# First expert's rows gathered by quarters and turned by VectorE, on one core of a Trainium2

## What is computed

```python
x = attention(q, k, v)                               # 2304 rows of 512
x = (sigmoid(x @ w_gate) * (x @ w_val)) @ w_out      # hidden size 1536
logits = x @ g + log1p(exp(x @ g_noise)) * noise     # 8 experts
top2, weight = two best experts of a row, softmax of the two
for e in range(8):                                   # hidden size 1024
    out[rows of e] += weight * (relu(x[rows of e] @ w1[e]) @ w2[e])
```

## Time and profile before

| | |
|---|---|
| median of 3 runs | 974.71 us (974.69 to 976.02) |
| the profiled execution | 974.4 us |
| its span, first to last instruction | 972.5 us |
| TensorE busy | 963.2 us, 99%, 6467 products |
| VectorE, ScalarE, GpSimd busy | 516.2, 372.1, 424.5 us |
| granted TensorE clock | 0.998 |
| the first expert's TensorE turns (L1097) | 20 transposes, 3.0 us busy |

### The profile page before, as it was taken

One profiled execution on the slowest core, in us unless ns is written; L12 is line 12 of the kernel. 1 busy time (PEld: TensorE's weight loads), 2 busy tenths in 40 slices (PEclk: granted clock), 3 DMA queues, 4 the chain that ended last, 5 costly groups with the idle time before them and its releaser, 6 DMA issues.

```text
span 972.5 us, 17622 instructions
## 1 busy us (share of the span) xinstructions
PE 963.2 (99%) x6467; PEld 847.9 (87%) x6467; DVE 516.2 (53%) x1285; ACT 372.1 (38%) x892; POOL 424.5 (44%) x417
## 2 busy tenths in 40 slices
PE   9999999999999999999999999999999999999997
PEld 7998888888888888888999899898998989898995
DVE  6565576765757576574546633444443434444430
ACT  6553343433333343422344423343434334343411
POOL 4882224242332434232215453664828284664402
PEclk9999999999999999999999999999999999999999
DMA  6756333343533325232134163672736465473503
GB/s 227 233 173 165 119 110 108 96 138 97 142 106 125 99 75 152 76 100 87 44 121 133 30 156 79 169 161 84 156 77 146 100 151 129 118 163 75 98 3 52
DMA packets 85335, 113.64 MB, mean 117 GB/s; under 512 B 20800, under 2 KB 48448, under 8 KB 85248
## 3 DMA queue, kind: packets, MB, share of 16 engines
q1 hardware_dynamic: 71376, 85.18, 30.0%
q0 software_dynamic: 13584, 27.05, 13.9%
q10 hardware_dynamic: 288, 0.26, 0.1%
HBM read 83.69 MB, written 28.77 MB: 116 GB/s over the span
## 4 chain that ended last, share of the span: by engine, by line
PE 98%; ACT 1%; DVE 0%; issue 0%; POOL 0%; POOLq 0%; DVEq 0%
PE bank L1129 22%; PE bank L1113 22%; PE bank L1018 16%; PE bank L1041 16%; PE bank L1024 11%; PE bank L1022 5%; PE bank L998 2%; PE bank L936 2%; PE bank L1136 1%; PE bank L1067 1%; PE bank L1077 0%; PE bank L954 0%; ACT arena L1268 0%; PE bank L1097 0%; POOL out L816 0%
## 5 line engine op out<-in xcount | busy, mean ns | idle before, releaser
L1024 PE MATMUL bank<-xr,wr 128*128 128x256 f32 x864 | 242.6, 281 | 0.0
L1018 PE MATMUL bank<-xr,wr 128*128 128x512 f32 x672 | 239.9, 397 | 0.0
L1113 PE MATMUL bank<-wr 128*128 128x256 f32 (+1 forms) x1536 | 223.4, 306 | 0.3 <-DVE wr L1748 0.3
L1113 PEld LDWEIGHTS bank<-wr 128*128 128x128 f32 x1536 | 221.2, 190 | 2.0 <-DVE wr L1748 0.7
L798 POOL DMA_INDIRECT arena<-x_rows,shared x128 | 139.8, 1092 | 131.2 <-DVE v_nat L1735 88.4
L763 POOL TENSOR_TENSOR hr<-arena,hr 128x256 fp32r<-128x256 f32 x84 | 62.0, 738 | 263.5 <-ACT hr L1319 263.5
L1041 PE MATMUL bank<-wr,hr 128*128 128x512 f32 x648 | 170.6, 398 | 0.0
L1024 PEld LDWEIGHTS bank<-xr,wr 128*128 128x128 f32 x864 | 163.6, 189 | 3.5
L1018 PEld LDWEIGHTS bank<-xr,wr 128*128 128x128 f32 x672 | 126.2, 188 | 30.2
L1041 PEld LDWEIGHTS bank<-wr,hr 128*128 128x128 f32 x648 | 114.0, 188 | 23.7 <-issue 0.6
L1129 PE MATMUL bank<-wr 128*128 128x512 f32 (+1 forms) x576 | 132.6, 390 | 0.0
(11 more groups left out here) (161 smaller groups left out, 1013.6 us busy)
## 6 DMA issues: line engine op xcount, KB each, us to landing
arena<-moe_w SPq DMA_DIRECT2D x36, 512.0 KB, 3.7
arena<-moe_w SPq DMA_DIRECT2D x112, 128.0 KB, 3.4
p_rows<-arena SPq DMA_DIRECT2D x28, 256.0 KB, 2.0
v_nat<-p_rows SPq DMA_DIRECT2D x112, 64.0 KB, 2.0
arena<-gv SPq DMA_DIRECT2D x12, 512.0 KB, 4.5
out<-zeros POOLq DMA_DIRECT2D x20, 256.0 KB, 2.8
x_rows<-arena SPq DMA_DIRECT2D x9, 512.0 KB, 3.9
arena<-k SPq DMA_DIRECT2D x17, 256.0 KB, 4.2
```

Source lines behind the costliest of these rows:

```text
L1018: pe.matmul(ps_g[m].rearrange("p (a n) -> p a n", a=2), gv_w[:, f, m, kk], xr[:, g % 2, :, kk], start=(kk == 0), stop=False, skip_group_ch ...
L1024: mm = pe.matmul(ps_g[m][:, 0:GT], gv_w[:, f, 2 + m, kk], xr[:, g % 2, 0, kk], start=False, stop=(kk == KC - 1), skip_group_check=True)
L1113: mm = pe.matmul(ps_h[u % 2][:, 0:n], w1_r[e % 2][:, a, kk, f * P:(f + 1) * P], xT[p][:, b, kk, 0:n], start=(kk + x == 0), stop=(kk == KC ...
```

## The change

It makes the first expert's tiles squared like all others. TensorE's `turn_g` goes, and its calls: three in slots 104 to 106 (n = 0, 1, 2) and two in `up(1, 0, f)` behind f = 4 and 6 (n = 6, 7). VectorE turns them: n = 0 at the end of slot 103, n = 1 in slot 104, n = 2 in slot 106, n = 6 behind f = 3, n = 7 behind f = 5. The high and low parts of n = 0, 1, 2 are made in slots 104, 105 and 107 (before: 104, 105, 106). GpSimd issues four DMAs for each of the five tiles. The first expert's w1 is loaded in quarters. The table `tab_q_first` holds both experts and takes eight DMAs; VectorE waits for it in slot 100 (before: slot 103). A new table `tab_q_next` for n = 6, 7 takes four DMAs ahead of `tab`; VectorE waits for it ahead of `hidden_low(1, 0, 0)`. `tab_q` holds all eight experts. Gather 7 is issued ahead of the second scatter. Apart from this, in the last group's choice `hidden_low(0, 0, 5)` stands behind the first three instructions rather than behind the first eight.

```diff
+    FIRST_ROWS = [LAST - 4, LAST - 3, LAST - 1]
...
-        def turned_at(n):
-
-            return x_t if squared(n) else ps_xt.rearrange("p (k m) -> p k m", k=KC)
...
         def gathers(n):
 
-            return 16 * sum(4 if squared(i) else 1 for i in range(n % 2, n + 1, 2))
+            return 64 * ((n - n % 2) // 2 + 1)
...
-                if n < KC and e >= SQUARES:
+                if n < KC:
 
                     for j in range(4):
                         sp.dma_start(raw[j * Q4:(j + 1) * Q4, n % 4], w1_q[e, j, n]).then_inc(raw_e[n % 4], 16)
...
-                    for j in range(4):
-                        sp.dma_start(tab_q_first[j * Q4:(j + 1) * Q4].rearrange("p b n w -> p b (n w)"),
-                                     places.rearrange("(b c e n) w -> c b e (n w)", b=4, c=Q4, e=NE)[:, :, SQUARES, 0:2 * HEAD]
-                                     ).then_inc(tab_q_first_in, 16)
+                    for e in range(AHEAD):
+                        for j in range(4):
+                            sp.dma_start(tab_q_first[j * Q4:(j + 1) * Q4, e].rearrange("p b n w -> p b (n w)"),
+                                         by_quarter[:, :, e, 0:2 * HEAD]).then_inc(tab_q_first_in, 16)
...
             sp.wait_ge(placed_late, 16 * 2 * CH * (GROUPS - EARLY))
+            for j in range(4):
+                sp.dma_start(tab_q_next[j * Q4:(j + 1) * Q4].rearrange("p b n w -> p b (n w)"),
+                             by_quarter[:, :, 0, 2 * HEAD:2 * TILES]).then_inc(tab_q_next_in, 16)
             sp.dma_start(tab[:].rearrange("p n w -> p (n w)"), places.rearrange("(p n) w -> p (n w)", p=P)).then_inc(tab_in, 16)
...
-                if n == AHEAD * HEAD:
-                    pool.wait_ge(tab_in, 16)
...
-                if squared(n):
-                    if n == HEAD:
-                        pool.wait_ge(quarters_first, 1)
...
+                if n == 0:
+                    pool.wait_ge(quarters_first, 1)
+                if n == AHEAD * HEAD:
+                    pool.wait_ge(quarters_next, 1)
+                if n == AHEAD * HEAD + LATE:
+                    pool.wait_ge(quarters_done, 1)
...
             gather(6)
+            gather(7)
             scatter(1)
-            gather(7)
             scatter(2)
...
-                if LAST - 4 <= s < LAST - 1:
-                    turn_g(s - (LAST - 4))
...
             for f in range(F2C):
                 up(1, 0, f)
-                if f in (4, 6):
-                    turn_g(f // 2 + 4)
...
-                if LAST - 4 <= s < LAST - 1:
-                    xt_high(s - (LAST - 4))
+                if s in FIRST_ROWS:
+                    xt_high(FIRST_ROWS.index(s))
...
                 relu(1, 0, f)
-                if f in (4, 6):
-                    xt_high(f // 2 + 4)
+                if f in (3, 5):
+                    xt_high(6 + (f - 3) // 2)
...
+                if s == LAST - 8:
+                    dve.wait_ge(tab_q_first_in, 16 * 4 * AHEAD)
+                    link(dve.tensor_scalar(quarter[:], quarter[:], 5, None, ALU.arith_shift_right))
+                    to_quarters(tab_q_first[:].rearrange("p e b n w -> p (e b n) w")[:, :, 0]).then_inc(quarters_first, 1)
                 if s == LAST - 5:
-                    dve.wait_ge(tab_q_first_in, 16 * 4)
...
-                if LAST - 4 <= s < LAST - 1:
-                    xt_low(s - (LAST - 4))
+                    turn_rows(0)
+                if s in FIRST_ROWS:
+                    xt_low(FIRST_ROWS.index(s))
+                if s == LAST - 4:
+                    turn_rows(1)
+                if s == LAST - 2:
+                    turn_rows(2)
...
             hidden_low(0, 0, 4)
-            choose_first(GROUPS - 1)
+
+            add_noise(GROUPS - 1)
             hidden_low(0, 0, 5)
+            choose(L[:], marks[:, 0], top[:, 0])
             choose_second(GROUPS - 1)
...
             low(1, HEAD)
+            dve.wait_ge(tab_q_next_in, 16 * 4)
+            to_quarters(tab_q_next[:].rearrange("p b n w -> p (b n) w")[:, :, 0]).then_inc(quarters_next, 1)
             for f in range(F2C):
                 hidden_low(1, 0, f)
...
-                if f in (4, 6):
-                    xt_low(f // 2 + 4)
+                if f == 3:
+                    turn_rows(6)
+                if f == 4:
+                    xt_low(6)
+                if f == 5:
+                    turn_rows(7)
+                    xt_low(7)
```

More of the change, by code:

```diff
@@ L135, in attention_two_moe_program @@
         noise_s = shared[:, 3 * WIN:].rearrange("p (t e) -> p t e", e=NE)
-        tab_q = shared[:, 0:8 * (NE - SQUARES) * TILES].bitcast(I32).rearrange("p (b e n w) -> p b e n w", b=4, n=TILES, w=2)
+        tab_q = shared[:, 0:8 * NE * TILES].bitcast(I32).rearrange("p (b e n w) -> p b e n w", b=4, n=TILES, w=2)
         zeros = sb("zeros", [P, P])
@@ L176, in attention_two_moe_program @@
         quarter = sb("quarter", [P, 1], I32)
-        tab_q_first = sb("tab_q_first", [P, 4, HEAD, 2], I32)
+        tab_q_first = sb("tab_q_first", [P, AHEAD, 4, HEAD, 2], I32)
+        tab_q_next = sb("tab_q_next", [P, 4, LATE, 2], I32)
         idx_r = sb("idx_r", [P, 1], I32)
@@ L350, in attention_two_moe_program @@
         quarters_first = sem("quarters_first")
+        tab_q_next_in = sem("tab_q_next_in")
+        quarters_next = sem("quarters_next")
         quarters_done = sem("quarters_done")
@@ L380, in attention_two_moe_program @@
         ORDER = [0, 1, 2, 5, 6, 7, 3, 4, 8, 9] + list(range(AHEAD * TILES, ALL))
-        def turned_at(n):
-            return x_t if squared(n) else ps_xt.rearrange("p (k m) -> p k m", k=KC)
         def turn_no(m):
             return ORDER.index(m)
-        def squared(n):
-            return ORDER[n] // TILES >= SQUARES
         def loads(q):
-            return 16 * sum(4 if i // UNITS >= SQUARES and i % UNITS < KC else 1 for i in range(q % 4, q + 1, 4))
+            return 16 * sum(4 if i % UNITS < KC else 1 for i in range(q % 4, q + 1, 4))
         def gathers(n):
-            return 16 * sum(4 if squared(i) else 1 for i in range(n % 2, n + 1, 2))
+            return 64 * ((n - n % 2) // 2 + 1)
         def is_early(m):
@@ L524, in _ @@
         def _(sp):
+            by_quarter = places.rearrange("(b c e n) w -> c b e (n w)", b=4, c=Q4, e=NE)
             def load_k(t):
@@ L788, in gather @@
                     pool.wait_ge(xt_turned, n - 1)
-                if squared(n):
-                    if n == HEAD:
-                        pool.wait_ge(quarters_first, 1)
[L792 to L800, removed]
-                pool.nop(nofuse=True)
-                pool.indirect_dma_start(x_g[:, n % 2], None, x2_rows[:, :], bass.IndirectOffsetOnAxis(row_no(m), 0)
-                                        ).then_inc(gathered[n % 2], 16)
+                if n == 0:
[4 more added lines that the diff above has]
+                    pool.wait_ge(quarters_done, 1)
+                pool.nop(nofuse=True)
+                e, a = divmod(m, TILES)
+                for b in range(4):
+                    if is_early(m):
+                        no = tab_q_first[:, e, b, a, 0:1]
+                    elif e == 0:
+                        no = tab_q_next[:, b, a - HEAD, 0:1]
+                    else:
+                        no = tab_q[:, b, e, a, 0:1]
+                    pool.indirect_dma_start(x_g[:, n % 2, b * P:(b + 1) * P], None, x2_quarters,
+                                            bass.IndirectOffsetOnAxis(no, 0)).then_inc(gathered[n % 2], 16)
             def scatter(m):
@@ L1089, in rank_rows @@
                 pe.matmul(ps_rank, tri[:], chosen[:], start=False, stop=True, skip_group_check=True).then_inc(ranked, 1)
[L1091 to L1098, removed]
             def up(e, p, f):
@@ L1383, in xt_high @@
                     act.wait_ge(hr_used, LAST)
-                act.copy(xT[p][:, 0, :, cols], turned_at(n)).then_inc(xt_hi, 1)
+                act.copy(xT[p][:, 0, :, cols], x_t).then_inc(xt_hi, 1)
             def relu(e, p, f):
@@ L1666, in choose_first, with add_noise @@
             def choose_first(g):
+                add_noise(g)
+                choose(L[:], marks[:, 0], top[:, 0])
+            def add_noise(g):
                 dve.wait_ge(soft, 3 * g + 2)
@@ L1731, in turn_rows @@
                 dve.wait_ge(gathered[n % 2], gathers(n))
-                dve.wait_ge(xt_hi, n)
-                dve.wait_ge(xt_lo, n)
+                if n:
+                    dve.wait_ge(xt_hi, n)
+                    dve.wait_ge(xt_lo, n)
                 dve.nop(nofuse=True)
@@ L1740, in xt_low @@
                 dve.wait_ge(xt_hi, n + 1)
-                dve.tensor_tensor(xT[p][:, 1, :, cols], turned_at(n),
+                dve.tensor_tensor(xT[p][:, 1, :, cols], x_t,
                                   xT[p][:, 0, :, cols].bitcast(F32), ALU.subtract).then_inc(xt_lo, 1)
```

9 lines of the change are left out of this document (1 added, 8 removed).

## The result

The changed kernel takes 978.59 us in the median of 13 runs (977.18 to 981.99), the kernel before 974.96 us in the 13 runs beside it (974.42 to 976.82). The ratio is 1.0036, with a 95% interval of 1.0029 to 1.0043: slower by 0.36%. I had forecast 976.2 us and a range up to 978.4, with the bound of "slower" at 976.66. The median lies 2.4 us above the forecast and 0.2 us outside the range.

The account below looks back on a forecast made before the run. TensorE was taken to bound the kernel (98% of the chain that ended last). Terms +1.7, -0.3 and +0.1 gave +1.5 us: 975.9 us for an execution like the profiled one, 976.2 as median, range 973.6 to 978.4.

Parts of the forecast that it names:

- Part 1: Turns of n = 0, 1, 2 moved to VectorE: -1.3 us of turns, +0.5 and +2.5 of TensorE waits, sum +1.7 us.
- the 2.5 us wait: TensorE waits 2.5 us at the first expert's first unit for VectorE's low part of n = 2.
- anything else: Remaining cases, such as a lower granted clock behind TensorE's first long wait; no size given, chance 0.03.
- Part 2: Hidden part 5 earlier inside the last group's choice removes TensorE's 0.34 us wait: -0.3 us.
- the bracket: The 0.34 us TensorE wait on VectorE behind the last group's choice, shown in the profile before.
- Part 3: Late tiles n = 6, 7: -0.9 us of turns, +1.0 of TensorE wait for the gather of n = 7, sum +0.1 us.
- the late gather decides: Rival: gather of n = 7 lands at 575.7, TensorE waits 3.7 us in place of 1.0; 978.9 us, chance 0.17.
- The covers: Part 1's extra gathers and tables, including VectorE's table wait in slot 100, are hidden behind other work: cost 0.
- The turns fit in: Rival: VectorE has unseen slack, so the waits of 0.5, 2.5 and 1.0 us go; 972.2 us, chance 0.10.
- A cheaper first part: Rival: the waits are half as long and the late gather lands at 571; 974.2 us, chance 0.15.
- GpSimd holds the low part of n = 2: Rival: GpSimd's gather issue blocks that VectorE instruction for 0.95 us, on the path to the first unit; 977.2 us, chance 0.05.

Follow-up runs that it names:

- experiment 3: Changed kernel with VectorE's turn and low part of n = 2 ahead of slots and weights of group 7, which move to slot 107; 975.82 us.
- experiment 4: Kernel before with only the high and low part of n = 2 moved from slot 106 to 107, TensorE still turning; 976.17 us.
- Experiment 2: Changed kernel with eight unused products of zeros on TensorE ahead of the first expert's first unit (the fill); 978.04 us.
- after: The changed kernel itself, with nothing else altered; 978.59 us.
- experiment 1: Kernel before with only the new order of the last group's choice; 974.17 us.
- experiment 6: Changed kernel with SyncE holding the second expert's last four weight units until gathers 7 and 8 have landed; 976.74 us.
- experiment 7: Changed kernel, weight loads held behind gathers 7 and 8, turn n = 6 behind f = 2, table conversion behind f = 4, gather 8 before both scatters; 975.8 us.
- experiment 5: Changed kernel with SyncE holding the second expert's last four weight units until gathers 6 and 7 have landed; 980.49 us.
- run without fill of the last session: The kernel of experiment 7 once more, in a later session where the kernel before took 988.34 us; 994.94 us.
- run with fill of the last session: The kernel of experiment 7 plus eight unused products of zeros ahead of the first unit, same later session; 996.1 us.

## Why the prediction was wrong, point by point

**Part 1, the path to the first unit: right.** Predicted -1.3, +0.5 and +2.5; measured -1.3, 0.43 and 2.14, and 1.6 for the sum of 1.7. VectorE's timeline has the chain that the prediction named, step by step:

```profile
521.71 0.38 DVE L1599 SCALAR_TENSOR_TENSOR arena<-arena,bank 128x256 f32<-128x256 f32 x1
522.56 0.43 DVE L1605 TENSOR_TENSOR hr<-arena,hr 128x256 fp32r<-128x256 f32 x1 [0.47 <-ACT hr L1303]
523.08 0.69 DVE L1729 TENSOR_TENSOR wr<-v_nat,wr 128x512 fp32r<-128x512 f32 x1
```

Hidden rows first, with ScalarE's high half between, then the low part of n = 2, done at 523.8. Experiments 3 and 4 show that its place in the list is the cause. One reading on the way was wrong without harm: "no gap stands between 510 and 520.8". Before, VectorE has two, of 0.47 us each, behind ScalarE's high half (at 512.69 and 517.05). The added turn did not fit into them, as they come from a wait for ScalarE: the mark for the ranking moved from 514.27 to 515.41, 0.9 us beyond the 0.3 by which this execution is later.

**What follows the long wait: wrong, and the first failed step.** The sum has nothing behind the 2.5 us wait; a lower clock stood only under "anything else", at 0.03. It cost 1.7 us in the profiled execution. What it cost in the median is less certain. Experiment 2 gives 0.55 us, which its runs can't tell from nothing. An estimate from experiment 3 gives about 1 us: its median is 2.8 below after's, while the two traces without the 1.7 us of clock differ by 1.4 from ranking to ranking and by 0.3 from there to `down(0, 3)`. TensorE has no wait over 0.34 us in this stretch of the kernel before, so none of my rows could tell what one of 2.5 us does to the clock. That was an operation without a row, and it needed a bound: half the clock over the next pieces of work (3.39 us between the starts of the first two units before) gives up to 3.4 us more.

**Part 2: right in kind, its term too small.** -0.6 in place of -0.3 (experiment 1), for the bracket.

**Part 3: the second failed step, its term mis-sized**, +1.9 in place of +0.1. "I put the landing just behind it, at 573": the turn that waited for it started at 577.61, which is 574.7 in the times of before (2.95 us less). GpSimd issued its last gather on the predicted beat, 571.21 (568.3, predicted 568.5). SyncE did not keep its own. The queue's rows, before and now:

```profile
559.15 10.43 SPq L680 DMA_DIRECT2D shared<-places  x16
569.63 2.14 SPq L592 DMA_DIRECT2D arena<-moe_w  x4
```

The sixteen table DMAs took 10.43 us in place of 8.14, so the loads began at 569.63 (566.7; predicted 564.5) and ran into the landing in place of ending ahead of it. I had priced them at the 8.14 us of a table that held seven experts; it now holds eight. All nine traces with the new tables have 10.41 to 10.44 us, also where the loads are held back, and the three with the old ones 8.14 to 8.33, so the longer time belongs to the changed kernel and not to one execution. By windows:

```profile
562.00:566.00 4.00, 4.00 (x26) 4.00 (x25) 0.54 (x1) 1.17 (x3) 2.92 (x3) 1.00 0.39 49
566.00:570.00 4.00, 4.00 (x26) 4.00 (x25) 1.08 (x2) 0.96 (x3) 2.91 (x4) 1.00 0.48 64
570.00:574.00 4.00, 3.78 (x23) 3.48 (x21) 1.89 (x4) 1.48 (x4) 3.39 (x3) 1.00 0.89 240
574.00:578.00 4.00, 3.80 (x23) 3.80 (x24) 1.59 (x4) 0.29 (x1) 3.08 (x4) 1.00 1.02 337
```

The DMA share, the last number but one of a row, was 1.00 from 562 to 572 us before; now it is 0.39 to 0.48 while GpSimd issues and 0.89 to 1.02 just as gather 7 is to land. The issue-to-landing time was 6.3 us at the worst. VectorE shows it:

```profile
577.61 0.71 DVE L1723 STREAM_TRANSPOSE v_nat<-arena 128x512 f32<-128x512 f32 x1 [2.41 <-DMA arena<-x_rows,tab_q_next]
```

From there to TensorE's unit at 580.34 are 2.7 us, as worked out (2.6). This is the rival "the late gather decides" at half its size: it had the landing at 575.7 and a wait of 3.7 us; the landing came at 574.7 and TensorE lost 1.86 us. That its 978.9 us lie beside the measured 978.6 is in part luck: the late tiles gave 1.8 us over the sum and not 2.7, and the clock, which this rival did not have, gave the rest. The wait of 0.42 us at 574.20 I had not foreseen. VectorE idles there until ScalarE is done, whose high part of n = 6 stands ahead of its relu; with the loads held back it is still 0.34 us (experiment 6), with the turn one unit earlier as well (experiment 7) it is gone. Experiments 5 to 7 show that the loads are what the gather meets. Why an eighth expert in the table costs SyncE 2.3 us was not tried.

**The covers: right.** The table wait in slot 100 was longer than nothing, and slot 101's product went 0.3 us behind the first instruction after it, at 494.41, where it stood at 492.58 before; no TensorE wait followed:

```profile
494.12 0.15 DVE L1802 TENSOR_SCALAR quarter<-quarter 128x1 int32<-128x1 int32 x1 [2.46 <-DMA tab_q_first<-places]
...
494.41 0.42 DVE L1599 SCALAR_TENSOR_TENSOR arena<-arena,bank 128x256 f32<-128x256 f32 x1
```

**The other rivals.** "The turns fit in" fell: the waits are there. "A cheaper first part" fell with them. "GpSimd holds the low part of n = 2" fell too: the instruction at 523.08 took 0.69 us, as in the 35 cases before, while GpSimd issued a gather:

```profile
522.53 0.95 POOL L799 DMA_INDIRECT arena<-x_rows,tab_q_first  x1 [3.05 <-DVE v_nat L1723]
```

An instruction held until GpSimd was done would have lasted past 523.5 + 0.69 us. The conflict does exist, the other way round: a gather that GpSimd starts while VectorE works on two inputs from SBUF is held. The low part of a weight unit (L1710, both inputs in SBUF) and a gather a moment later:

```profile
516.18 1.22 DVE L1710 TENSOR_TENSOR wr<-arena,wr 128x1024 fp32r<-128x1024 f32 x1
516.22 2.00 POOL L799 DMA_INDIRECT arena<-x_rows,tab_q_first  x1 [0.30 <-issue]
```

The issue took 2.00 us in place of 0.95 and ended 0.82 us behind VectorE's instruction. From 480 to 960 us, 36 gathers of this trace start under such an instruction that is listed by itself; all end 0.81 to 0.85 us behind it. So of the Trainium skill, SBUF — State Buffer, section "Who interferes with whom", the rule on two inputs in SBUF held where GpSimd came second, and did not show where VectorE came second, in the pair at 523.08. The rival had the order in which it costs nothing here.

**What stays open.** Why the clock falls in some executions and not in others behind the same 2.14 us, and not behind 1.86 us at 580.34 or 2.38 us at 586.98 in experiment 5. The two traces with the fill have no fall at the first unit, and four of the five with the long wait unfilled have one; so few traces make the fill's effect likely and do not prove it, and no set of runs shows its worth in the median.

## What to carry to other kernels

Work moved from a full engine to an emptier one pays only if the receiving engine's list has room at that point: ask of each consumer what stands ahead of it in the list, and move the step, not the load; here moves of a few lines turned +0.36% into -0.18% (the late loads, held back, are a part of it). When a gather is split or moved later, follow every bulk load that SyncE will issue meanwhile, and hold it behind all the gathers that matter, not the first. And give a new wait of TensorE that is as long as those behind which the clock fell here (2.0 to 4.0 us) a second price, its clock: 1.7 us where the fall came, nothing where it did not.

## What the runs showed of the hardware

- Behind a TensorE wait of 2.14 or 2.15 us the granted clock was 0.50 for some 3.4 us in four profiled executions (after, 5, 6, and the run without fill of the last session) and 1.00 in one (7); it cost 1.6 to 1.7 us. It also fell behind waits of 2.00 us (experiment 3, start of the kernel), 2.75, 2.94 and 2.65 us (the run with fill of the last session, at 535.74, 578.74 and 597.65) and 4.00 us (the run without, at 602.39). It did not fall behind 0.78, 1.86 and 2.38 us, shown above, nor behind 2.07 us (the run without fill, at 579.24). So waits of 2.0 to 2.4 us stand on both sides.
- GpSimd's issue of a gather took 0.95 us in the median and up to 2.00 us when it began under a VectorE instruction with both inputs in SBUF; it then ended 0.81 to 0.85 us behind that instruction (36 cases in after's trace).
- A gather by quarters landed between 2.7 and 6.3 us after its issue among the eight issued from 562 to 572 us, with the DMA share between 0.39 and 1.02.
- The kernel before took 974.9 to 975.0 us beside all other runs and 988.3 us in the last session, and kernel 7, whose tiles come in by many small DMAs, lost more there (1.0085 against 1.0008). That the small DMAs are the reason is a guess.
